# Reordering the prologue of a fused recurrence and two-stage MLP kernel: loads, weight splits and the second triangular inverse

## The reference, cut to what matters

```python
def _attn_ref(q, k, v, beta):                       # B, H, S, D = 4, 8, 768, 48
    k_n = k / (norm(k, axis=-1) + 1e-6)
    for t in range(S):                              # state: B, H, D, D
        y[:, :, t] = einsum('bhd,bhde->bhe', q[:, :, t], state)
        v_old = einsum('bhde,bhd->bhe', state, kt)
        state = state + bt * einsum('bhd,bhe->bhde', kt, vt - v_old)

x = y.transpose(0, 2, 1, 3).reshape(3072, 384)
h = x @ w_in; g = maximum(0.01 * h, h); x = g @ w_out        # d_ff = 2048
# then 8 experts (d_ff 1024): tokens with x @ w_skip > 0 go to argmax(x @ w_gate)
out = x + gate_w * (maximum(x @ w1[e], 0) @ w2[e])           # for those tokens
```

## Time and profile before

| | us |
|---|---|
| three runs | 895.62, 896.46, 896.35 (median 896.35) |
| the profiled execution | 895.62, its span 893.9 |
| TensorE busy | 774.3 (87%) |
| VectorE busy | 663.7 (74%) |
| ScalarE busy | 495.5 (55%) |
| GpSimd busy | 416.3 (47%) |
| mean granted clock of TensorE | 0.976 of full |

### The profile page before, as it was taken

One profiled execution on the slowest core, in us unless ns is written; L12 is line 12 of the kernel. 1 busy time (PEld: TensorE's weight loads), 2 busy tenths in 40 slices (PEclk: granted clock), 3 DMA queues, 4 the chain that ended last, 5 costly groups with the idle time before them and its releaser, 6 DMA issues.

```text
span 893.9 us, 27698 instructions
## 1 busy us (share of the span) xinstructions
PE 774.3 (87%) x10782; PEld 624.0 (70%) x10783; DVE 663.7 (74%) x1334; ACT 495.5 (55%) x1108; POOL 416.3 (47%) x498
## 2 busy tenths in 40 slices
PE   0123679999999999999999999999999899999985
PEld 0123558787777777777778788878777668778764
DVE  6485978888888888788888887866868873563382
ACT  5435555767576766666675766554464652441261
POOL 5213163627262635445453634352353665564473
PEclk9996599999999999999999999999999999999998
DMA  9489748577778777766768676347516765263100
GB/s 224 107 196 194 137 75 140 103 141 139 138 142 139 137 124 133 139 126 131 135 121 145 103 140 123 76 70 232 176 20 205 248 234 182 84 204 118 44 17 17
DMA packets 357277, 119.76 MB, mean 134 GB/s; under 512 B 330450, under 2 KB 348420, under 8 KB 356784
## 3 DMA queue, kind: packets, MB, share of 16 engines
q1 hardware_dynamic: 351424, 104.33, 55.9%
q0 software_dynamic: 3232, 7.64, 2.5%
q10 hardware_dynamic: 2512, 6.29, 2.0%
HBM read 63.53 MB, written 21.25 MB: 95 GB/s over the span
## 4 chain that ended last, share of the span: by engine, by line
PE 32%; DVE 24%; issue 11%; DMA 11%; ACT 11%; SPq 6%; POOL 4%; DVEq 0%; POOLq 0%; ACTq 0%
PE b_acc L849 8%; PE b_h L836 6%; PE b_h L743 6%; PE b_acc L756 6%; DVE stage L1485 4%; SPq L498 4%; DVE inv L1411 3%; DMA t_dram<-inv 3%; PE b_ch L682 3%; DVE inv L1417 3%; DMA natq<-x_dram,id_in 3%; ACT ga L954 2%; DMA operands<-t_dram 2%; ACT operands L954 2%; ACT stage L1074 2%
## 5 line engine op out<-in xcount | busy, mean ns | idle before, releaser
L1910 POOL TENSOR_TENSOR stage<-stage 128x256 f16<-128x256 f32 x192 | 142.7, 743 | 252.9 <-ACT stage L954 252.1
L743 PE MATMUL b_h<-stage,wt 128*128 128x256 f16 x1728 | 221.7, 274 | 11.2 <-DVE stage L1344 9.1
L756 PE MATMUL b_acc<-wt,stage 128*128 128x384 f16 x1152 | 218.4, 326 | 4.3 <-POOL stage L1910 3.4
L743 PEld LDWEIGHTS b_h<-stage,wt 128*128 128x128 f16 x1728 | 158.9, 98 | 31.6 <-DVE stage L1344 10.9
L756 PEld LDWEIGHTS b_acc<-wt,stage 128*128 128x128 f16 x1152 | 106.7, 97 | 59.1 <-POOL stage L1910 6.6
L954 ACT ACTIVATE stage<-stage 128x256 f16<-128x256 f32 x192 | 80.0, 417 | 106.4 <-DVE stage L1485 105.5
L1485 DVE SCALAR_TENSOR_TENSOR stage<-b_h,stage 128x256 f32<-128x256 f32 x192 | 80.8, 421 | 43.2 <-ACT stage L1074 41.6
L849 PE MATMUL b_acc<-wt,operands 128*128 128x384 f16 x552 | 97.3, 326 | 7.6 <-DVE operands L1525 7.6
L836 PEld LDWEIGHTS b_h<-y,wt 128*128 128x128 f16 x1656 | 93.5, 98 | 6.6 <-issue 4.7
L836 PE MATMUL b_h<-y,wt 128*128 128x128 f16 x1656 | 96.5, 219 | 1.6 <-DVE y L1344 0.7
L1417 DVE TENSOR_REDUCE inv<-inv 128x30 f32<-128x90 f32 (+4 forms) x180 | 85.1, 473 | 5.8
(11 more groups left out here) (215 smaller groups left out, 1292.9 us busy)
## 6 DMA issues: line engine op xcount, KB each, us to landing
operands<-in_moe_w_dram SPq DMA_DIRECT2D x18, 1536.0 KB, 7.5
a_sys<-a_dram SPq DMA_DIRECT2D x24, 256.0 KB, 4.3
kc<-operands SPq DMA_DIRECT2D x22, 256.0 KB, 4.1
natq<-in_q_dram SPq DMA_DIRECT2D x24, 192.0 KB, 3.9
raw_v<-in_v_dram SPq DMA_DIRECT2D x24, 192.0 KB, 4.2
stage<-y SPq DMA_DIRECT2D x96, 48.0 KB, 2.0
x_dram<-stage SPq DMA_DIRECT2D x24, 192.0 KB, 2.9
out_dram<-stage SPq DMA_DIRECT2D x24, 192.0 KB, 3.3
```

Source lines behind the costliest of these rows:

```text
L743: mm = pe.matmul(b_h[f % 2][:, 0:GT], wt[0][:, a, d * FF + f * P:d * FF + (f + 1) * P], xT[:, g % 2, b, d, :], start=(i == 0), stop=(i == ...
L756: mm = pe.matmul(b_acc[w][:, 0:DM], g16[:, f % 4, a, w * P:(w + 1) * P], wt[1][:, b, f * DM:(f + 1) * DM], start=(f == 0 and (a, b) == PAR ...
L1910: pool.tensor_tensor(g16[:, f % 4, LO, :], g32[:, f % 4, :], g16[:, f % 4, HI, :], ALU.subtract).then_inc(g_lo, 1)
```

## The change

- SyncE: load_v(0) and load_k(2) move behind compact_k(1). inverse_out(0) moves behind blocks_out(1), and inverse_back(0) behind blocks_back(1). load_q(1) and the loads of the gate weights now come ahead of blocks_out(1).
- w_out is loaded as 4 and 12 of its 16 pieces, not 8 and 8. ScalarE issues the first piece right after the load of w_in's third part, and the second after a wait for the transposes of q(0).
- ScalarE: split_w_in(2) moves ahead of q_high(0); gram_out(1) ahead of squares(2), and squares(2) and inverse_high(0) stand behind it; first_z follows inverse_high(0). q_high(1), the high half of the gate weights and the splits of the quarters 2 and 3 of w_out move out of turn(0) to the end of the prologue.
- VectorE: split_w_in(2) moves ahead of q_low(0), norm_sum(2) ahead of scan_z_low(0). In turn(0) the quarters 1, 2, 3 of w_out are split at f = 2, 3, 4 (before: 1, 6, 7) and q_low(1) comes at f = 5, 6 (before: 3, 4). SECOND has 19 links in f = 0 to 7 as before, but 8 of them in f = 0 and 1.

```diff
-        SECOND = (0, 0, 0, 5, 4, 4, 4, 2, 0, 0, 6, 8, 0, 0, 0, 0)
+        SECOND = (5, 3, 3, 1, 2, 3, 2, 0, 0, 0, 6, 8, 0, 0, 0, 0)
...
             turn_k(0)
-            load_v(0)
             blocks_out(0)
             blocks_back(0)
-            load_k(2)
             turn_k(1)
             turn_q(0)
             compact_k(1)
-            inverse_out(0)
-            inverse_back(0)
-            blocks_out(1)
+            load_v(0)
+            load_k(2)
             load_q(1)
...
+            blocks_out(1)
+            inverse_out(0)
             blocks_back(1)
+            inverse_back(0)
...
-                f = (slice(0, FT // 2), slice(FT // 2, FT))[h]
+                f = (slice(0, 4), slice(4, FT))[h]
...
             def split_w_out(i):
-                act.wait_ge(w_out_loaded[i // 2], 16)
+                if i < 2:
+                    act.wait_ge(w_out_loaded[i], 16)
...
-                    if g == 0 and f in (2, 3):
-                        q_high(1, f - 2)
-                    if g == 0 and f in (5, 6):
-                        split_w_out(f - 3)
-                    if g == 0 and f == 7:
-                        act.wait_ge(wg_loaded, 32)
-                        copy(wg16[:, HI], wg[:], GW_S).then_inc(wg_hi, 1)
...
             load_w_in(2, 3)
+            load_w_out(0)
             split_w_in(1)
             for st in range(B):
                 gram_out(0, st)
             a21_high(0)
+            split_w_in(2)
             for x in range(2):
                 q_high(0, x)
             act.wait_ge(const_pool, 1)
             seed(0)
-            act.wait_ge(a_loaded[0], 32)
-            load_w_out(0)
-            split_w_in(2)
-            squares(2)
-            first_z()
-            inverse_high(0)
-            root(2)
+            act.wait_ge(q_turned, 32)
+            load_w_out(1)
             for st in range(B):
                 gram_out(1, st)
+            squares(2)
+            inverse_high(0)
+            first_z()
+            root(2)
             for st in range(2):
                 p_high(0, st)
...
             split_w_out(0)
+            for x in range(2):
+                q_high(1, x)
+            act.wait_ge(wg_loaded, 32)
+            copy(wg16[:, HI], wg[:], GW_S).then_inc(wg_hi, 1)
             seed(1)
-            split_w_out(1)
-            act.wait_ge(t_loaded, 128)
-            load_w_out(1)
+            for i in range(1, 4):
+                split_w_out(i)
...
-                    if g == 0 and f == 1:
+                    if g == 0 and f in (3, 4):
+                        split_w_out(f - 1)
+                    if g == 0 and f in (5, 6):
+                        q_low(1, f - 5)
+                    if g == 0 and f == 2:
                         split_w_out(1)
-                    if g == 0 and f in (3, 4):
-                        q_low(1, f - 3)
-                    if g == 0 and f in (6, 7):
-                        split_w_out(f - 4)
...
             a21_low(0)
+            split_w_in(2)
             for x in range(2):
                 q_low(0, x)
             inverse(0, 0, LINKS)
             inverse_low(0)
+            norm_sum(2)
             for r in range(2):
                 scan_z_low(0, r)
-            norm_sum(2)
             norm(2)
-            split_w_in(2)
```

## The result

The changed kernel took 902.17 us (median of 5 runs, 900.58 to 902.89) against 895.62 us for the kernel before in the same comparison: ratio 1.0066, 95% interval 1.0049 to 1.0084. It is slower by 0.66%, about 6 us. Four more executions on record outside this comparison, the profiled one among them, took 899.37 to 900.52 us: slower than before too, but by 4 to 5 us. The forecast was 900.7 us with a range to 903.5. The profiled execution of the changed kernel took 900.34 us, with a span of 898.6 us (before: 893.9). The total work is the same: here is the busy time of each engine from the page of the kernel after.

What follows compares the result with a forecast made beforehand. Bound: chain of waits before the loop, from the Gram blocks' memory round trip to the first up matmul at 105.50. Sum 64 + 5.5 + 18.1 + (25.7 - 3.3) = 110.0, 4.5 us slower: 900.7 us, range 893.8 to 903.5.

Steps and rivals of the forecast that it cites:

- The Gram wait stays: Gram blocks' round trip through memory: the 8.86 us wait remains, last Gram write reported near 38.0.
- Rival B: The 8.86 us Gram wait goes with load_v, later times 6.6 us earlier: 894.2 us, chance 0.12.
- The transposes end earlier: Transposes of k(1) and q(0): 5.9 us earlier, the last at 50.6 instead of 56.6.
- L, the landing of load_k(2): Time load_k(2), which squares(2) needs, lands beside w_out: 64, bounds 57 to 66; faster than before only if before 59.5.
- From L to N, the end of norm(2): From load_k(2)'s landing through squares(2) and the work behind it to norm(2)'s end: 5.5 us, ending at 69.5.
- From N to the first scan copy: From norm(2)'s end to ScalarE's first scan copy: 18.1 us against 16.7, copy at 87.6.
- The stretch to the first up matmul: From first scan copy to first up matmul: 3.3 us shorter than 25.7, ends 1.5 and 4.5, through early second-inverse links.
- The sum: First up matmul at 110.0 against 105.50, 4.5 us slower.
- The shift kept to the end: After the first up matmul: a constant shift to the end; the prediction is wrong if it is not kept.
- Rival A: load_k(2) hardly held by w_out, landing at 57 to 58: 2 us faster, 894.3 us, chance 0.17.
- Rival C: No difference: w_out, v and k bytes all pass at 370 GB/s, load_k(2) lands at 60.1: 897 us, chance 0.10.
- D: Worse than forecast: load_k(2) lands at 66 and the stretch gains only 1.5: 904.6 us, chance 0.06.

Runs made afterwards that it cites:

- the sixth run: Changed kernel with load_k(2) back at its old place ahead of turn_k(1), load_v(0) still late, against the kernel before: 903.31 us, ratio 1.0081.
- the second run: Changed kernel with the old portions SECOND = (0, 0, 0, 5, 4, 4, 4, 2, ...) for the second inverse, against the kernel before: 907.16 us, ratio 1.0122.
- the fourth: Kernel before, with GpSimd's 0.5 KB write going to a tile in on-chip memory instead of DRAM: 889.37 us, ratio 0.9934.
- the first experiment: Changed kernel with ScalarE's second load of w_out (2.36 MB) issued after squares(2), against the kernel before: 894.32 us, ratio 0.9975.
- the third run: Kernel before, with GpSimd's 0.5 KB write to memory issued at about 6.5 us instead of 28.26: 892.79 us, ratio 0.9966.

## Why the prediction was right, step by step

- **The Gram wait stays.** Forecast near 38.0, measured 37.65 (29.11 + 8.54). Rival B, that load_v held it, is refuted, and the tiny write is shown to be the cause by two runs.
- **The transposes end earlier.** Forecast 50.6; ScalarE, which waits for them, issued w_out at 51.34, so they ended some 0.7 us later than forecast. compact_k(1) was issued at 48.53, near the 49.1 of the forecast, but TensorE started on it at 57.23 instead of 53.7. The forecast let w_out hold load_v and load_k(2) and left out that compact_k(1) was in flight beside it too. It cost nothing here, because squares(2) was later still; in the sixth run it became the bound.
- **L, the landing of load_k(2).** This was the term that decided the sign: forecast 64, with 57 to 66 as ends; measured 65.65. w_out itself was faster than scaled from its halves (10.5 us after issue, not 11.7 to 13.7), and the small loads were held for its whole length; what the forecast lacked was that SyncE's queue is held as well: with 7.68 us for two issues, the second load_k(2) is only issued at 58.09, not by 53.4. That 64 comes so near is in part luck, since two errors of opposite sign meet in it.
- **From L to N, the end of norm(2).** Forecast L + 5.5, measured 71.00, which is L + 5.35. nat_k(2) on GpSimd took 1.47 us, forecast 1.5, against the 3.38 of the earlier trace rows.
- **From N to the first scan copy.** Forecast 18.1 us, measured 17.9 (88.90).
- **The stretch to the first up matmul.** Forecast 22.4 us, measured 22.5, and its gain is confirmed by the second run in sign and roughly in size (4.6 us by that run, just over the forecast's upper end of 4.5).
- **The sum.** Forecast +4.5 us at the first up matmul, measured +5.9. Of the 1.4 missed, L gives 1.65 and all else -0.3. Of the terms of the sum only this one was off by more than 0.2. Some roundings of the prediction don't agree with each other (50.8 + 9.2 is 60.0, not 60.1; the last transpose moves from 56.6 to 50.6, 6.0 us and not 5.9; 18.1 against 16.7 is 1.4, not 1.5; 900.8 became 900.7); none touches the outcome.
- **The shift kept to the end.** Not as forecast: the prediction wanted a constant shift and named its loss as a sign of being wrong. The sign is kept, a fifth of the size is lost. Here is one pass of the same matmuls late in the loop, from TensorE's timelines of the kernel after; that of the kernel before starts at 632.88.

```profile
637.33 1.16 PE L743 MATMUL b_h<-stage,wt 128*128 128x256 f16 x9 [1.19 <-DVE stage L1342]
```

At that point it is 4.5 us, and 4.7 at the end of the span. It was 5.9 us at the first up matmul and is 5.5 to 6.1 where each of the next seven groups starts; it drops by 1.2 between the eighth and the ninth (446 to 495 us). Between the first up matmul and the matmul shown here the other eight kernels drift too against the profile of the kernel before, by -2.0 (the second experiment) to +1.8 us (the fourth), so the drop is nothing special to this change; its cause is open. That the 4.7 us at the end lie so near the 4.5 of the forecast is luck: 5.9 arrived at the loop and 1.2 got lost. The medians differ by 6.5 us.

Rival A (load_k(2) hardly held, faster by 2 us) did not happen, but the first experiment made it: without w_out beside it the load takes 4.2 us and the kernel is at 0.9975. Rival C (all bytes at one common rate, L = 60.1) fails twice: the rate isn't shared by bytes, w_out had ten parts in eleven of it, and it isn't kept, since from 61 to 65 us, with w_out through and only small loads left, it was 162 to 195 GB/s instead of 370. D's landing at 66 nearly came, its lost stretch did not.

## What to carry to other kernels

A large load issued beside small ones that someone waits for strikes whichever of them is in flight, through their data and through the issuing queue; put it behind the last wait of that kind, not just behind the transfer that used to suffer (in the three runs with w_out behind squares(2) it still struck the second group's Gram writes). When a wait on a DMA can't be explained by bytes, look for a tiny write to memory issued just before it, and change its target rather than its place. An engine that works in order passes a wait to everything queued behind it: before a late load is moved, see what stands behind its consumer and needs nothing of it.

## What the runs showed that I had not expected

- A 0.5 KB write to memory delays by several us the reports of DMAs that end behind it: up to 8.5 and 8.9 us instead of 1.9 for 64 KB writes, and in the third run 11.2 instead of 4.7 us for a load of k and 14.7 instead of 10.1 for the loads of q. Writes reported ahead of it are not touched. Aimed at the chip's own memory it delays nothing that can be seen, and the kernel gains 0.66%.
- Two queues passed equal numbers of packets (1416 and 1387) of unequal size: the small loads of 192 KB took 7.5 to 10.9 us beside the large one, against about 4 us without it.
- The issue of such a load is slow too: 7.68 us of SyncE's queue for two, against 1.35.
